# Four-way butterflies and a feature sum moved within a fused attention, Fourier and MLP kernel

## The reference

```python
# 1 decayed linear attention (blocks of tokens, running 64x64 state per head)
out = (q k^T * Dmask) v + (q * lam_pow) state
# 2 Fourier mixing, layer norm, MLP (512 -> 2048 -> 512)
mixed = real(fft(fft(x, axis=1), axis=2)); u = x + mixed
un = (u - mean(u)) / sqrt(var(u) + 1e-6)
x = u + relu(un @ w_ch1) @ w_ch2
# 3 gated projection
gate = sigmoid(causal_conv5(x)); y = (gate * (x @ w_val)) @ w_out
```

## Time and profile before

| | |
|---|---|
| times of three runs | 444.06, 446.07, 446.08 us (median 446.07) |
| profiled execution | 448.07 us, of which the span is 446.3 us |
| TensorE busy | 432.3 us (97%) |
| VectorE, ScalarE, GpSimd busy | 262.0 (59%), 150.1 (34%), 144.0 us (32%) |
| attention and Fourier, batch 0 | about 0 to 88 us |
| MLP of both batches and, beside it, Fourier of batch 1 | about 88 to 375 us, then the projections |

### The profile page before, as it was taken

The page is one execution under the profiler, slowest core; times in us unless marked ns, Lnnn a source line. Parts: engine busy times, 40 slices in busy tenths (PEclk is TensorE's granted clock), DMA queues, the critical chain, the costliest instruction groups (busy, mean ns, idle before and its releaser), DMA issues.

```text
span 446.3 us, 7167 instructions
## 1 busy us (share of the span) xinstructions
PE 432.3 (97%) x2934; PEld 412.5 (92%) x2934; DVE 262.0 (59%) x433; ACT 150.1 (34%) x284; POOL 144.0 (32%) x97
## 2 busy tenths in 40 slices
PE   8699989899999999999999999999999999999997
PEld 8588779799999999999999999999999999889985
DVE  2455997967248835364433327948557548999220
ACT  1144442382223411113441236362233243515221
POOL 1434332259323322422647223234224252400000
PEclk9899999999999999999999999999999999999999
DMA  6958720222022020302202202103202110001112
GB/s 197 352 205 278 233 99 2 94 95 95 7 90 94 1 94 1 94 1 95 96 0 95 94 1 94 62 34 95 58 37 94 53 42 2 1 1 71 72 47 94
DMA packets 13889, 36.52 MB, mean 82 GB/s; under 512 B 1561, under 2 KB 3105, under 8 KB 13857
## 3 DMA queue, kind: packets, MB, share of 16 engines
q1 hardware_dynamic: 13856, 36.07, 24.2%
HBM read 32.91 MB, written 3.15 MB: 81 GB/s over the span
## 4 chain that ended last, share of the span: by engine, by line
PE 84%; DVE 9%; DMA 3%; issue 1%; ACT 1%; SPq 1%; DVEq 0%
PE ps L532 10%; PE ps L534 10%; PE ps L555 10%; PE ps L554 10%; PE ps L533 10%; PE ps L553 10%; PE ps L644 2%; PE ps L643 2%; PE ps L642 2%; PE ps L621 2%; DMA chunks<-in_qkv 2%; PE ps L622 2%; PE ps L623 2%; PE ps L406 2%; PE ps L433 2%
## 5 line engine op out<-in xcount | busy, mean ns | idle before, releaser
L728 ACT ACTIVATE hh<-ps 128x384 fp32r<-128x384 f32 x64 | 31.5, 493 | 176.7 <-PE ps L534 176.7
L992 DVE SCALAR_TENSOR_TENSOR hl<-ps,hh 128x384 fp32r<-128x384 f32 x64 | 35.3, 556 | 87.0 <-ACT hh L728 87.0
L532 PE MATMUL ps<-cen_h,w1h_a 128*128 128x384 f32 x128 | 43.9, 343 | 0.5 <-DVE hl L992 0.5
L532 PE MATMUL ps<-cen_h,w1h_b 128*128 128x384 f32 x128 | 44.2, 345 | 0.0
L534 PE MATMUL ps<-cen_h,w1l_b 128*128 128x384 f32 x128 | 43.1, 337 | 0.0
L555 PE MATMUL ps<-hh,w2l_b 128*128 128x384 f32 x128 | 43.1, 337 | 0.0
L534 PE MATMUL ps<-cen_h,w1l_a 128*128 128x384 f32 x128 | 43.1, 337 | 0.0
L554 PE MATMUL ps<-hl,w2h_b 128*128 128x384 f32 x128 | 43.1, 337 | 0.0
L533 PE MATMUL ps<-cen_l,w1h_a 128*128 128x384 f32 x128 | 43.1, 337 | 0.0
L553 PE MATMUL ps<-hh,w2h_b 128*128 128x384 f32 x128 | 43.1, 337 | 0.0
L533 PE MATMUL ps<-cen_l,w1h_b 128*128 128x384 f32 x128 | 43.0, 336 | 0.0
(11 more groups left out here) (161 smaller groups left out, 1006.5 us busy)
## 6 DMA issues: line engine op xcount, KB each, us to landing
raw_a<-in_mlp SPq DMA_DIRECT2D x16, 512.0 KB, 4.7
raw_b<-in_mlp SPq DMA_DIRECT2D x16, 512.0 KB, 4.4
chunks<-in_qkv SPq DMA_DIRECT2D x12, 512.0 KB, 6.0
chunks<-in_qkv SPq DMA_DIRECT2D x22, 256.0 KB, 6.0
out<-out_sb SPq DMA_DIRECT2D x12, 256.0 KB, 2.0
raw_a<-in_val SPq DMA_DIRECT2D x2, 512.0 KB, 4.5
raw_b<-in_out SPq DMA_DIRECT2D x2, 512.0 KB, 4.5
seq_c<-const_seq SPq DMA_DIRECT2D x1, 768.0 KB, 6.0
```

The source lines that it names most:

```text
L532: mm(bank, wh_, xh, start=r == 0, stop=False)
L728: nc.scalar.activation(hh[:, slot, j], ps[j][:, 0:TB], ACT.Relu).then_inc(s_hh, 1)
L992: stt(hl[:, slot, j], ps[j][:, 0:TB], 0.0, hh[:, slot, j].bitcast(F32), ALU.max, ALU.subtract).then_inc(s_hl, 1)
```

## The change

Three edits, all of them in the order of instructions; no computation is changed.

- VectorE: `radix4(6)` goes behind `add_pair(0, 0)`; `radix4(8)` goes ahead of `add_pair(0, 2)`; `radix4(9)` goes from behind `hidden_sum(0, 3)` to ahead of `add_pair(0, 3)`. `radix4(7)` stays first after the mask and the fold of its turn.
- GpSimd: the second feature sum, `hidden_sum(0, 2)`, waits for all four instructions of `radix4(9)` besides what it waited for.
- ScalarE: the two ReLUs of the MLP's first step go ahead of `spectrum_copy(8)` and `spectrum_copy(9)`.

```diff
@@ ScalarE
             cen_hi(0, 1)
+            hidden_hi(steps[0])
             spectrum_copy(NC + 2)
             spectrum_copy(NC + 3)
-            hidden_hi(steps[0])
             squares(0, 0)
@@ VectorE
                 if n == N - 3:
+                    add_pair(0, 0)
                     radix4(NC)
-                    add_pair(0, 0)
                     add_pair(0, 1)
                 if n == N - 2:
                     radix4(NC + 1)
+                    radix4(NC + 2)
                     add_pair(0, 2)
-                    radix4(NC + 2)
+                    radix4(NC + 3)
                     add_pair(0, 3)
             hidden_sum(0, 3, nc.vector, dve)
-            radix4(NC + 3)
@@ GpSimd
             hidden_sum(0, 1, nc.gpsimd, pool)
+
+            pool.wait_ge(s_r4, R4 * (NC + 4))
             hidden_sum(0, 2, nc.gpsimd, pool)
```

## The result

The changed kernel takes 444.23 us against 446.89 (medians of 22 runs each, taken side by side); the ratio is 0.9931, with a 95% interval from 0.9908 to 0.9954, so 2.1 to 4.1 us, and 3.1 in the middle. Its profiled execution has a span of 442.1 us, 4.2 less than before. Not all of that is the change: in this execution the loads of the input chunks held TensorE for 2.0 + 0.4 us where they had held it for 2.7 + 2.0 us, and the stretch that the change touches begins 0.90 us sooner. From here on I measure from the start of chunk 10's mask (L870, at 61.45 us before and 60.55 us after) to the first matmul of the MLP's third hidden product, and call this the distance. It is 103.08 - 61.45 = 41.63 us before and 98.83 - 60.55 = 38.28 us after: 3.35 us less.

What follows compares the result with a forecast made beforehand. TensorE alone bounds 104 to 420 us; some 3.6 us of waiting lie before, at 60 to 104. Gains 1.57 + 1.15 + 0.63 = 3.35 us off 446.07 give 442.7 us; range 441.9 to 444.4 with two rivals, about 8 in 10.

Steps and rivals of the forecast that it cites:

- two rivals: GpSimd's sum and fourth addition exclude each other: gain 1.4 us, chance 0.13; ReLU edit pays nothing: 2.72 us, chance 0.15.
- 1a: second pair sooner: First addition ahead of chunk 6's butterfly: TensorE's wait before its second pair nearly goes, 1.57 us gained.
- 1b: the mean sooner beyond that: Chunks 8 and 9 moved, GpSimd waiting: VectorE's third sum starts 2.72 us sooner, 1.15 us of it from this part.
- 3: from the mean to the third hidden product: ReLUs ahead of the spectrum copies: TensorE's wait at the second hidden product goes, 0.63 us gained, bounds 0.46 to 0.80.
- chunk 7's L892, longer by: VectorE's butterfly instruction beside GpSimd's first sum, ending near 72.68 us: a stall larger by 0.6 us than before.
- third addition, after the mask: VectorE, behind chunk 8's butterfly: starts at 74.42 us, 0.37 us late to its data but 1.20 us ahead of before.
- wait left at the mean: TensorE reaches the mean at 81.39 us, the mean starts at 81.73 us: some 0.3 us of wait left from 1.49.
- cover of the low weights: GpSimd's low part ends at 102.04 us, TensorE wants it at 102.45 us for the third hidden product: 0.4 us.
- GpSimd's wait: GpSimd's second sum waits for chunk 9's butterfly, avoiding a VectorE stall; ends at 80.05 us with 0.65 us of cover.
- beside PSUM additions alone: GpSimd's second sum, 78.1 to 80.05 us, overlaps only additions with one PSUM input; no slowdown was counted.
- The slower rival: Group 1's low weights come late at the third hidden product; slower than before from 3.75 us of delay; chance 0.06.
- The steps of 2.0 us in the times: Measured runs stand at 444.06, 446.07, 448.07 us, so 442.06 or, less likely, 444.06 us would be read.

## Why the prediction was right

The forecast, 442.7 us in a range from 441.9 to 444.4, stood on 3.35 us of gain; the measured time of 444.23 us lies in the range, and the ratio's 3.1 us (2.1 to 4.1) holds the gain. That the time itself lies in the range is in part luck. It is outside the 441.9 to 443.5 that the forecast had for its own mechanism, in the part that was added for two rivals, and neither of these came true. The sum started from 446.07, the median of the three runs then known, while the 22 runs have 446.89; from there 3.35 us less is 443.54. The other 0.7 us are within the spread of the runs: the medians differ by 2.66 us, where the ratio's estimate is 3.1 and the trace has 3.35.

The mechanism is right. Against its steps, with times from chunk 10's mask:

| step | forecast | trace after |
|---|---|---|
| 1a: second pair sooner | 1.57 us | 4.65 - 3.12 = 1.53 us |
| 1b: the mean sooner beyond that | 1.15 us | 2.65 - 1.53 = 1.12 us |
| 3: from the mean to the third hidden product | 0.63 us | 18.63 - 17.93 = 0.70 us |
| chunk 7's L892, longer by | 0.6 us | 1.14 - 0.63 = 0.51 us |
| third addition, after the mask | 12.97 us | 73.66 - 60.55 = 13.11 us |
| wait left at the mean | 0.3 us | 0.37 us |
| cover of the low weights | 0.4 us | 98.83 - (96.18 + 2.40) = 0.25 us |

It came out because each of the three gains was read as a bracket of TensorE, and each was followed up to what is late next. That the parts add was shown by running each alone. Two small errors cancelled on the way: the third addition starts 0.14 us later after the mask than reckoned, but its halves start 74.86 - 73.66 = 1.20 us apart, not 1.34. (They are 1.34 apart when the second half waits for TensorE, as it did at 75.62 us.)

Three things in it were wrong:

- *GpSimd's wait.* I had an instruction with two SBUF inputs always stand still beside the sum. Without the wait L895, 0.17 us behind the sum, went first in three executions of three with chunk 9 there. The step "beside PSUM additions alone" is right, but it earns nothing.
- *The slower rival's price.* I charged one microsecond for each of delay past the cover, so that the gain would be lost from 3.75 us of delay on, and left the clock out. With the low weights late it was 2.67 us of distance and 1.34 more behind it, where the clock had fallen.
- *The steps of 2.0 us in the times.* I took them for the grain of the measurement. The 22 runs lie anywhere from 441.75 to 447.27 us. The granted clock groups them better. Of 52 runs of the kernel before (two above 452 us left out) and 34 of the changed one in these comparisons (not all side by side), those with a mean clock of 1.00 average 445.42 us (18 runs) and 442.20 us (12 runs): 3.2 us, the forecast nearly to the tenth. Those at 0.996 average 446.79 (22) and 444.57 us (16), those near 0.992 448.52 (12) and 446.60 us (6).

## What to carry to other kernels

Where one engine is the bound, look for its few brackets, and for each ask what the releasing engine did just before that nobody was waiting for; move that work behind something that waits anyway, and work out the new cover of everything that slides. Before adding a wait against a collision, run the order without it: which side yields may not be the one seen in the trace. Parts worth a microsecond in 440 are read from one profile between two fixed points, with the granted clock between them beside it, and from times only if these are sorted by granted clock.

## What the runs showed of the hardware

An instruction of VectorE with two SBUF inputs and a two-input sum of GpSimd excluded each other wherever they met in these rows, and at the same spacing either may be the one to stand still (2.04 us for L895 against 0.41, or 2.67 us for the sum against 1.82). An instruction with one input in PSUM and the sum pass freely side by side (1.31 us for the addition, 1.82 us for the sum).

The clock can fall from 2.4 to 1.2 GHz at quite short waits of TensorE, which the prediction left out. In the stretch that I measure it did so in each of the three runs in which TensorE waited 2.35, 2.57 or 2.76 us, and in one of three profiled executions with the 1.62 us wait for the first addition; it didn't at any of the 1.49 us waits at the mean (three profiles). The length of a wait doesn't settle it: in the kernel before, the clock stayed at 1.00 for 5 us behind a 2.71 us wait for a chunk load,

```profile
13.21 0.69 PE L418 MATMUL ps<-chunks,kd 128*64 128x64 f32 x16 [2.71 <-DMA chunks<-in_qkv]
```

```profile
13.00:18.00 5.00, 2.83 (x50) 2.43 (x50) 2.95 (x6) 1.65 (x5) 2.20 (x2) 1.00 1.04 373
```

and what else decides isn't shown. One fall cost 1.34 us (low weights late) and 1.60 us (ReLUs alone) where it could be measured by itself; with chunk 8 behind the third addition, the way from the mean to the third hidden product became longer by 2.70 us, and with the buffers exchanged as well by 100.38 - 81.29 - 17.93 = 1.16 us. Removing a short wait can thus be worth more than its length, though here the share of runs with a full clock was alike, 18 of 52 and 12 of 34: in the profiles most falls come earlier, while TensorE waits for the chunk loads.
